# An early expert block beside the routing, and an expert loop turned by one tile

## The reference

```python
mask = q_bucket[:, :, :, None] == k_bucket[:, :, None, :]
attn = softmax(where(mask, scale * q @ k.T, -1e9));  x = attn @ v          # [1536, 512]
logits = x @ w_gate + modality_bias[modality_id];  e_idx = argmax(logits)
out[e_idx == e] = gate_w * (relu(x[e_idx == e] @ w1[e]) @ w2[e])           # 512 -> 1024 -> 512
h = out @ w_in;  g = max(h, 0) + alpha * min(h, 0);  return g @ w_out      # 512 -> 2048 -> 512
```

## Time and profile before

| | |
|---|---|
| median of 3 runs | 728.23 us (728.03 to 729.34) |
| the profiled execution | 728.45 us, of it 726.6 us span |
| PE busy | 696.6 us, 96% of the span |
| DVE / ACT / POOL busy | 474.6 / 356.8 / 218.2 us |
| end of attention, last fold's matmuls | 268.84 us |
| first matmul of expert block 0 | 288.12 us |
| first matmul of expert block 1 | 312.03 us |
| first matmul of the dense network | 451.25 us |

### The profile page before, as it was taken

The page is one execution under the profiler, slowest core; times in us unless marked ns, Lnnn a source line. Parts: engine busy times, 40 slices in busy tenths (PEclk is TensorE's granted clock), DMA queues, the critical chain, the costliest instruction groups (busy, mean ns, idle before and its releaser), DMA issues.

```text
span 726.6 us, 12149 instructions
## 1 busy us (share of the span) xinstructions
PE 696.6 (96%) x4071; PEld 617.1 (85%) x4072; DVE 474.6 (65%) x884; ACT 356.8 (49%) x686; POOL 218.2 (30%) x305
## 2 busy tenths in 40 slices
PE   6999999999999975999999999999999999999995
PEld 4899999999999963999899997788888888888884
DVE  6898989999998858620144213766667666766662
ACT  3788878878888842421152223333343333433331
POOL 6656455555555524300111152300007000010002
PEclk9999999999999996999999999999999999999998
DMA  7975856648362006798111122000003000010001
GB/s 152 249 209 142 207 166 150 184 119 229 120 151 68 23 23 225 221 355 299 58 58 43 37 93 72 15 0 0 0 0 116 0 0 0 1 58 0 0 1 58
DMA packets 40061, 70.93 MB, mean 98 GB/s; under 512 B 7180, under 2 KB 19164, under 8 KB 39508
## 3 DMA queue, kind: packets, MB, share of 16 engines
q1 hardware_dynamic: 32484, 55.01, 26.9%
q0 software_dynamic: 3472, 10.55, 4.9%
q10 hardware_dynamic: 4064, 4.85, 2.1%
HBM read 33.98 MB, written 16.78 MB: 70 GB/s over the span
## 4 chain that ended last, share of the span: by engine, by line
PE 90%; DVE 4%; issue 2%; ACT 1%; DMA 1%; POOL 1%; POOLq 0%; ACTq 0%; DVEq 0%; SPq 0%
PE bank L823 8%; PE bank L1002 6%; PE bank L992 6%; PE bank L994 6%; PE bank L993 6%; PE bank L1004 6%; PE bank L1003 6%; PE bank L807 4%; PE bank L842 4%; PE bank L808 4%; PE bank L844 4%; PE bank L921 4%; PE bank L923 4%; PE bank L922 4%; PE bank L947 3%; PE bank L943 3%
## 5 line engine op out<-in xcount | busy, mean ns | idle before, releaser
L1073 ACT ACTIVATE probs<-bank,raffine 128x768 f32<-128x768 f32 x96 | 95.5, 995 | 39.6 <-DVE raffine L1296 39.6
L1290 DVE TENSOR_REDUCE rmin<-bank 128x1 f32<-128x768 f32 x96 | 91.4, 952 | 9.4 <-PE bank L808 8.6
L706 POOL DMA_INDIRECT out<-o_sb,token_s x12 | 12.1, 1010 | 238.6 <-ACT o_sb L1228 158.4
L823 PE MATMUL bank<-cst,probs 128*128 128x128 f32 x576 | 81.5, 276 | 2.1 <-DVE pt_lo L1304 1.9
L1567 DVE SCALAR_TENSOR_TENSOR ht_lo<-bank,ht_hi 128x512 fp32r<-128x512 f32 x28 | 19.0, 690 | 98.1 <-ACT ht_hi L1160 98.0
L823 PEld LDWEIGHTS bank<-cst,probs 128*128 128x128 f32 x576 | 67.9, 141 | 10.8 <-issue 5.8
L1304 DVE TENSOR_TENSOR pt_lo<-bank,pt_hi 128x384 fp32r<-128x384 f32 x128 | 70.3, 553 | 10.2 <-ACT pt_hi L1090 8.9
L992 PE MATMUL bank<-x_hi,wi_hi 128*128 128x512 f32 (+1 forms) x196 | 75.8, 387 | 0.7 <-DVE x_lo L1599 0.7
L1002 PE MATMUL bank<-wo_hi,g_hi 128*128 128x512 f32 x192 | 75.1, 391 | 1.3 <-DVE g_lo L1618 1.3
L1181 ACT ACTIVATE wi_hi<-ff_raw 128x512 fp32r (+1 forms) x48 | 30.4, 633 | 92.9 <-PE bank L994 91.9
L993 PE MATMUL bank<-x_lo,wi_hi 128*128 128x512 f32 (+1 forms) x196 | 75.4, 385 | 0.0
(11 more groups left out here) (223 smaller groups left out, 1625.4 us busy)
## 6 DMA issues: line engine op xcount, KB each, us to landing
w_raw<-in_moe_w SPq DMA_DIRECT2D x8, 1024.0 KB, 11.9
y_slots<-zeros SPq DMA_DIRECT2D x13, 512.0 KB, 4.4
ak<-k_his SPq DMA_DIRECT2D x28, 192.0 KB, 3.6
ff_raw<-in_moe_w_in SPq DMA_DIRECT2D x4, 1024.0 KB, 11.1
ff_raw<-in_moe_w_out SPq DMA_DIRECT2D x4, 1024.0 KB, 12.8
y_slots<-y_sb ACTq DMA_DIRECT2D x14, 256.0 KB, 2.1
aq<-q_los SPq DMA_DIRECT2D x16, 192.0 KB, 3.7
v_raw<-in_v SPq DMA_DIRECT2D x16, 192.0 KB, 3.6
```

The lines of the kernel that those rows point to most:

```text
L823: mm = pe.transpose(lane[1 + hf][:, t * P:t * P + P], probs[:, m % 3, kt * P:kt * P + P], C["ident"])
L1073: act.activation(probs[:, m % 3, :].rearrange("p (a c) -> p a c", a=2), s_ps[m % 2], ACT.Exp, bias=raffine[:, col, 1:2], scale=raffine[:, ...
```

## The change

After step 56 of attention, when batch 0's logits are complete, the kernel finds out which expert has most of batch 0's tokens and takes its first 256 of them as an extra first block. DVE does that in some 40 small operations strewn over steps 56 to 90 (`early`), PE in 13 small matmuls at steps 62, 71 and 77. SP loads the expert's `w1` in eight chunks of 256 KB, POOL splits them (`split_chunk`) and gathers the rows after step 79; PE turns them at steps 84 and 85, with the split of ACT and DVE behind. `w2` of that expert is loaded when the last scores are made; ACT splits the high parts after its loop, and POOL takes the remainders. PE computes the block (`first_block`) right after the last fold, with the routing's own matmuls inside: the counts after a third of the up product, the index after it, the next block's transposes in the middle of the second down tile. The chosen tokens are taken out of the later routing (`first_pos`, `first_place`, `one_hot` times `upper`).

The loop over the other blocks starts at 1 and is turned by one tile: the second down tile of a block is computed at the head of the next turn, the last one behind the dense network's first transposes. Two duties move between queues: the dense network's weights are issued by ACT behind `block(1)`, no longer by SP, and the parts for the sort wait for a `place_done` that now comes after the splits of block 1. `keep_warm` ahead of block 0 goes, and so does the one ahead of the dense network where the last tile is a full one. Some tiles move in memory; the zeroing of `y_slots` is 14 transfers in the first four pairs instead of 13 over seven.

```diff
+        if CHUNK_STEP <= n < CHUNK_STEP + 3 * CHUNKS and (n - CHUNK_STEP) % 3 == 0:
+            split_chunk((n - CHUNK_STEP) // 3)
+        if n == INDEX_STEP + 2:
+            pool.wait_ge(early_read, 3)
+            pool.wait_ge(x_stored, 16 * KD)
+            for tt in range(BT):
+                pool.indirect_dma_start(
+                    xg[:, tt, :], None, x_dram[0:SEQ], bass.IndirectOffsetOnAxis(idx_first[:, tt:tt + 1], 0)
+                ).then_inc(rows_in[tt], 16)
...
+    def split_chunk(c):
+        at = (slice(None), c // 2, slice(c % 2 * 512, c % 2 * 512 + 512))
+        pool.wait_ge(w1e_in, 16 * (c + 1))
+        pool.tensor_copy(w1e_hi[at], w1e_raw[:]).then_inc(w1e_hi_done, 1)
+        pool.wait_ge(w1e_hi_done, c + 1)
+        pool.tensor_tensor(w1e_lo[at], w1e_raw[:], w1e_hi[at], ALU.subtract).then_inc(w1e_ready, 1)
...
+    for hf in range(2):
+        cs = slice(hf * 4, hf * 4 + 4)
+        pool.wait_ge(w2_hi_done[hf], 1)
+        pool.tensor_tensor(w2_lo[:, cs], w2_raw[:, cs], w2_hi[:, cs], ALU.subtract).then_inc(w2_ready[hf], 1)
     pool.wait_ge(idx_ready, 1)
...
-    pe.wait_ge(part_ready, 1)
...
-    keep_warm(WARM[1], 7)
...
-    turn_rows(0)
-    keep_warm(WARM[5], 7)
+    def first_block():
+        pe.wait_ge(w1e_ready, CHUNKS)
+        pe.wait_ge(bx_lo, BT)
+        for fc in range(FC):
+...
+            if fc == 2:
+                route_counts()
+        route_index()
+        down_tile(0, 0, 0)
+        down_tile(0, 0, 1, between=4)
...
-    block(0)
-    with pe.Fori(1, n_blocks) as i:
-        block(i)
+    first_block()
+    block(1)
+    with pe.Fori(2, n_blocks) as i:
+        second_tile(i - 1)
+        block(i)
...
     turn_tiles(0, range(GT))
-    keep_warm(WARM[2], 5)
+    second_tile(n_blocks - 1, last=True)
...
+    block(1)
+    act.wait_ge(sort_made, 1)
+    for part in range(2 * KD):
+        load_ff(part)
+    with act.Fori(2, n_blocks) as i:
+        store_second(i)
...
+        block(i)
```

More of the change, by code:

```diff
@@ L907, in _ @@
-            turn_rows(0)
-            keep_warm(WARM[5], 7)
-            pe.wait_ge(table_ready, 1)
-            n_blocks = pe.value_load(table[0:1, TB_NB:TB_NB + 1], min_val=1, max_val=NBMAX)
+                    for no, made in enumerate((COUNT_STEP, RANK_STEP, INDEX_STEP)):
+                        if n == made + 1:
+                            pe.wait_ge(early_read, no + 1)
+                    if n == COUNT_STEP:
+                        pe.wait_ge(part0_ready, 1)
+                        pe.matmul(early_ps, ones_b[:], part0_b[:], start=True, stop=True).then_inc(count0_made, 1)
@@ new lines, in block, with down_tile @@
+                down_tile(i, u, 0)
+            def down_tile(i, u, tt, between=None):
+                ts = slice(tt * P, tt * P + P)
+                if tt == 0:
+                    pe.wait_ge(y_out, BT * i + 1)
+                for fc in range(FC):
+                    if fc == between:
+                        pe.wait_ge(rank_read, 1)
+                        for nxt in range(BT):
+                            turn_rows(1, nxt, bank[:, 4 + nxt, :])
+                    if tt == 0 and fc % 4 == 0:
+                        pe.wait_ge(w2_ready[fc // 4], u + 1)
+                    if tt == 0 and fc % 2 == 0:
+                        pe.wait_ge(h_lo, 4 * i + fc // 2 + 1)
+                    pe.matmul(bank[:, 6 + tt, :], ht_hi[:, fc, ts], w2_hi[:, fc, :],
+                              start=(fc == 0), stop=False)
+                    pe.matmul(bank[:, 6 + tt, :], ht_hi[:, fc, ts], w2_lo[:, fc, :],
+                              start=False, stop=False)
+                    mm = pe.matmul(bank[:, 6 + tt, :], ht_lo[:, fc, ts], w2_hi[:, fc, :],
+                                   start=False, stop=(fc == FC - 1))
+                mm.then_inc(y_made, 1)
@@ L1163, in _, with block @@
+            store_first(0)
+            for tt in range(BT):
+                split_rows(1, tt, bank[:, 4 + tt, :])
+            def block(i):
+                u = act.value_load(table[0:1, bass.ds(i + (TB_U - 1), 1)], min_val=1, max_val=E)
+                switch = act.value_load(table[0:1, bass.ds(i + (TB_SW - 1), 1)], min_val=0, max_val=1)
+                hidden(i)
                 with act.If(switch > 0):
                     split_w1(u + 1, (0,))
-                split_rows(i + 1)
+                for tt in range(BT):
+                    split_rows(i + 1, tt, bank[:, 4 + tt, :])
@@ L1533, in _, with hidden @@
-            n_blocks = dve.value_load(table[0:1, TB_NB:TB_NB + 1], min_val=1, max_val=NBMAX)
-            split_w1(0, (0,))
-            split_rows(0)
+            def hidden(i, parts=range(FC // 2)):
+                for fp in parts:
+                    dve.wait_ge(h_hi, 4 * i + fp + 1)
+                    dve.scalar_tensor_tensor(ht_lo[:, 2 * fp:2 * fp + 2, :],
+                                             bank[:, fp, :].rearrange("p (a t) -> p a t", a=2), 0.0,
+                                             ht_hi[:, 2 * fp:2 * fp + 2, :], ALU.max, ALU.subtract
+                                             ).then_inc(h_lo, 1)
@@ L1579, in block @@
                     split_w2(u + 1)
-            block(0)
-            with dve.Fori(1, n_blocks) as i:
+            block(1)
+            with dve.Fori(2, n_blocks) as i:
                 block(i)
```

549 lines of the change are left out of this document (364 added, 185 removed).

## The result

The changed kernel takes 740.23 us, the median of four runs (738.65 to 742.84); the kernel before took 728.57 beside it. The ratio is 1.0163, with a 95% interval of 1.0130 to 1.0196: slower by 1.6%. The profiled execution took 739.34 us.

What follows compares the result with a forecast made beforehand. The prediction took PE, busy 96% of the span, as the bound, so all gain was a matter of waits. Five terms, 5 - 8.2 + 4.5 + 8.5 - 2.6, gave +7.2 us, hence 735 us, range 719 to 743.

Steps and rivals of the forecast that it cites:

- B: Last fold to block 1's first matmul: -8.2 us, a gain cut by POOL's two w_lo delaying DVE's routing chain.
- D: Dense network's eight loads on ACT: +8.5 us, their issue delays block 2's hidden rows and the clock falls.
- A: Work added in attention: +5 us, mostly from DVE and POOL blocking each other.
- C: Rows of block 2: +4.5 us, their gather comes late behind the splits of block 1 and blocked POOL work.
- E: Last tile: -2.6 us, its down work covers the split before the dense network's first matmul.
- The first rival: Ports do not hold DVE up across the routing: B -18.2, C at most 1, time 722 us; 1 in 5.
- The rival in which ACT's queue takes the loads at once: ACT's queue swallows the dense network's loads: D is nothing, time 727 us; 3 in 20.
- The last rival: Attention pays in full, DVE the bound: A is 12 us, time 742 us; 1 in 10.

Runs made afterwards that it cites:

- e5: The changed kernel with POOL's split of the early expert's eight w1 chunks cut to 8 of 512 elements each; 737.51 us, ratio 1.0125.
- e9: e6 with each of POOL's eight w1e_lo subtractions inside attention cut into four of 128 elements; 714.70 us, ratio 0.9802.
- e7: The changed kernel with row_hot0 in three parts over steps 74 to 76 and first_place's three instructions moved behind cplace; 740.37 us, ratio 1.0167.
- e1: The changed kernel with the early block's two w2_lo subtractions moved from POOL to VectorE; 734.09 us, ratio 1.0060.
- e3: The changed kernel with block 2's rows gathered on POOL before it makes the sort's operands; 733.97 us, ratio 1.0062.
- e6: The changed kernel with the edits of e1, e2 and e3 together; 716.51 us, ratio 0.9842.
- e2: The changed kernel with the eight loads of the dense network's weights issued by SP again; 733.40 us, ratio 1.0062.
- e4: The changed kernel with TensorE multiplying the last block's second tile before the transposes of the dense network's first rows; 741.31 us, ratio 1.0161.
- e10: e4 with ScalarE also copying and storing the last tile before splitting the dense network's first weights and rows; 744.06 us, ratio 1.0206.
- e1b: The changed kernel with each of POOL's two w2_lo subtractions cut into four of 512 elements, still on POOL; 738.85 us, ratio 1.0137.

## Why the prediction was right

It said slower, by 7.2 us on the profiled execution, through five terms. Each term has the sign that it named, and each is larger than said. The causes of B and D were named in full, that of A in part, those of C and E by half; C, D and E lie outside the bounds given for them (6, 11 and -3), D and E by little.

**A, +5 against +6.1.** That VectorE and POOL block each other was right, and the value lay between the bounds. What e5 and e9 add is the split: 2.0 us go when POOL's chunks are cut away and 2.3 when only its long subtraction is cut into pieces; the rest stays without it. How the rest divides between VectorE's own additions and their waits for POOL's old `pt_lo` was not settled: e7 moved some of it and gained nothing. At 204.35, before the first chunk is subtracted, the added `in_first`, 6 elements, takes 0.98 us beside a `pt_lo` of POOL.

**B, -8.2 against -10.7.** The wait came where it was put, with POOL's two subtractions at 4.5 us instead of the 4.6 worked out, and e1 shows that they are its cause. The size was off in three places. The counts came 11.1 us after the fold, not 12.0. Counts and ranks took 0.7, not 0.9. The 60 matmuls behind them took 295.14 - 286.68 = 8.5 us, not 7.2 + 2.4: the clock was back at about 289.3, 3.3 us after the matmuls resumed instead of the 4.8 read from the earlier trace rows. The Trainium skill (SBUF — State Buffer, Who interferes with whom) says that the engine that came first holds the shared pair of ports for the whole instruction; the 4.41 and 4.42 us of `dlt` and `key`, and 1.11 and 1.22 when POOL's instruction is a quarter as long, agree with it. The first rival, which let VectorE slip through, is out.

**C, +4.5 against +7.3.** The rows came 4.0 us late, within the bounds and near the value. What failed is a step that was left out: the clock falls behind this wait too. It was costed in B and D and not here; e3 shows it as 3.3 us in this profile, and the others give 1.8 to 3.2. The working also added up short: its own parts (0.6, some 6, up to 6.3, 2.3 and 3.9) come to 19 us at the upper end, not 18. The rows were there at 15.3.

**D, +8.5 against +11.3.** The issues took less than on SP, 17.5 us instead of 20.5. The 2.4 us from ACT's last issue to PE were mis-sized: `y_sb` starts 0.2 us after it, the store takes 3.23 us behind the loads and not 0.39, and from there to `ht_hi` ACT spends 2.8 us, most of it on the four table loads at the head of a turn, L1333, L1334, L1305 and L1306 in the chain (2.9 us in e6, with no transfer of the dense net in its way). With `ht_hi` and `ht_lo` it is 8.3 us. So PE waited 9.10, not 6.0, and the clock cost 2.2, near the 2.4 said. e2 confirms the cause. The rival in which ACT's queue takes the loads at once is out.

**E, -2.6 against -3.5.** The mechanism was half of it. The tile does cover the split, and the dense net's first matmul follows it with no wait; by e4 that is worth 1.4 us. The larger part, 2.1 us, lies between e4 and the kernel before, where ACT puts the last copy and store ahead of its first splits. e10 shows 1.4 of it as ACT's order; the rest is mixed with the zeros that the change drops and was not tested. The prediction did not look at ACT's order.

The last rival, attention paying 12 us, is out as well: no profiled execution shows over 6.6. That the net result came within 3.7 us is in part luck, because the errors have both signs: +1.1, -2.5, +2.8, +2.8, -0.9 sum to 3.3, and the sort's 0.5 was in no term. With their sizes alone they come to 10.1.

The change itself was not a loss in its idea. The stretch from the last fold to block 1's first matmul goes from 43.2 to 27.8 us once VectorE is let through, and both hold a whole block of work. What cost more were three placements in queues, each mended by moving lines.

## What to carry to other kernels

When work is moved under another stage, list for every engine what its queue now has in front of the step that the next stage waits for; here a 4.5 us subtraction, seven small products and eight loads each stood ahead of something urgent, and cost 4 to 11 us apiece. Price a wait of TensorE with the clock behind it (in the changed kernel's profile 1.3, 3.3 and 2.2 us behind waits of 6.7, 4.0 and 9.1), not by its length alone. Read the same stretch in every profile whose edit lies elsewhere before a difference of a microsecond is explained. Undo suspects together as well as one by one: e2 alone looked like 7 us because its loads met a gather that e3 moves away.

## What the hardware showed that was not expected

- The granted clock was at half behind a wait of 3.20 + 0.81 us for rows (0.50 from 327 to 330), in e1b behind one of 3.95 (0.50 from 296 to 298) and in e10 behind one of 2.23 (0.54 from 467 to 469). It stayed at 1.00 behind 1.63 in e1b, 1.60 in e1 and 1.42 in e6.
- A store of 256 KB issued behind eight loads of 1 MB on the same queue held ACT for 3.23 us instead of 0.34. The eight issues took 0.62 to 4.63 us each, and the loads landed 6.3 to 14.5 us after their issue.
- The same POOL subtraction took 4.52 us for 2048 elements in one instruction and 5.04 in four; for 512, 1.28 in one and 1.83 in four. VectorE's waits shrank with the piece all the same.
- An operation on 6 elements took VectorE 0.98 us, a cast of 12 took POOL 1.80: what set the time was the instruction that the other engine had under way.
- Large loads that start with a gather delay it: in e2 the gather began as early as in the changed kernel, and TensorE waited 7.29 us for its rows instead of 4.01.
- The first 40 us vary by up to 3.6 us from one execution to the next. Whoever compares attention between two profiles has to take that off first.
